# Value tiles in three overlapped steps, later roundings of the weights' sums, and one tile's taps behind x

## The chip, the cores and the metric

The kernel runs on one core of a Trainium2 chip. Such a core has five engines with a queue each: TensorE (PE in the profile; its weight loads are PEld) multiplies, VectorE (DVE), ScalarE (ACT) and GpSimd (POOL) compute elementwise, and SyncE (SP) issues the transfers here. The engines run on their own and meet at semaphores. The metric is the device time of one execution in microseconds, given as the median over runs.

## The reference

Sparse attention feeds a feed-forward block with a convolution gate, which feeds a block with a spatial gate. The change lies at the seam of the last two.

```python
# B, S = 2, 768; 512 model features, 1024 inner features
x = attention(q, k, v)                         # (B, S, 512)

h = np.maximum(x @ w_in, 0.0)                  # first layer
conv_out = sum(conv_w[k] * shifted(h, k - 1) for k in range(3))   # "taps"
gate = 1.0 / (1.0 + np.exp(-conv_out))
x = h * gate @ w_out                           # second layer

h = np.maximum(x @ w_in2, 0.0)                 # third layer
u, v = h[..., :512], h[..., 512:]              # gate halves and value tiles
v_n = (v - mean(v)) / np.sqrt(var(v) + 1e-6)   # over the 512 features of a row
v_s = einsum("ts,bsd->btd", w_spatial, v_n) + b_spatial[None, :, None]
out = (u * v_s) @ w_out2
```

## The kernel before

All products run in fp32 split in two: each operand X is held as a rounded part X_hi and a remainder X_lo = X - X_hi, and each product is three matmuls (hi x hi, hi x lo, lo x hi). ScalarE makes the rounded parts, VectorE the remainders. So nearly every tile that TensorE takes has a rounding on ScalarE and, behind it, a subtraction on VectorE.

The program is written out engine by engine. Each engine's instructions are issued in the order of the code, and a wait on a semaphore holds up everything behind it on that engine. Nothing schedules the work but this order. The stages of the changed stretch, in the order of TensorE's work (b is the batch, 0 or 1; halves c are of the 768 columns):

1. Second layer of batch 0: eight x tiles x2 (`second_layer`), four for each half. Tile n and tile n + 4 share a bank, so TensorE waits for `x2_lo_in` (VectorE's `rest_of_x2(n)`, L1461) before tile n + 4. Beside it VectorE computes taps, gate products and remainders of batch 1: `taps(3, m)` are two operations (L1433, L1438) on tile m of its second half, whose first tap ScalarE has made (L1006).
2. Value tiles of batch 0: six tiles of 128 rows x 512 features (`value_half`), twelve matmuls each, in banks 4 to 7. For tile j ScalarE does `relu_v(j)` (L1044, out of the bank into a ring `vr` of VR = 3 rows), VectorE `row_stats(j)` (L1559, L1561), GpSimd `invert_std(j)` (L842, L845), VectorE `normalise_v(j)` (L1566), ScalarE `round_v(j)` (L1049), VectorE `rest_of_v(j)` (L1572). `relu_v(j)` for j of 3 and more waits for `v_lo_in`, which `rest_of_v(j - 3)` raises. In between ScalarE does sigmoids (L998) and roundings `round_g` (L1003) of batch 1 and VectorE gate products `gate` (L1447).
3. Gate halves of batch 0: eight groups of twelve matmuls (`gate_half`) in banks 0 to 3. ScalarE's `relu_u(n)` (L1055) empties a bank, and TensorE waits for it (`left_u`) before group n + 4.
4. Second layer of batch 1 (`second_layer_by_halves`) in Strassen's form with seven passes of 24 matmuls: X, Y, R, then one that adds onto X (L2139), V, another that adds (L2139), Z. It needs sums of weight blocks (`sum_f2_s`, L1512 to L1520; their roundings `round_f2_s` on ScalarE, L1011; their remainders `rest_of_f2_s` on VectorE, L1527) and differences of activation blocks (`sum_f2_t`, L1495; `rest_of_f2_t`, L1502). X needs g11_lo (L1467); Y needs g21_lo (`rest_of_g21`, L1472); R needs the sum 4 and g22_lo (L1477); the first adding pass needs the sum 2, the difference t2 and "c11" (`sum_f2`, L1548). The differences t overwrite the raw activations, and `rest_of_g21` and what follows write into the place of x2; VectorE therefore waits for `u_done` (all gate halves of batch 0 computed) before `rest_of_g21`.
5. Value tiles and gate halves of batch 1, then the spatial product and the output.

In the second batch VectorE already runs the value tiles as `row_stats(s)`, `normalise_v(s - 1)`, `rest_of_v(s - 2)`; there `vr` has a row for each tile.

Of the kernel before, what the change touches and what calls it, by code (L numbers as in the profile page):

```python
# [15 lines left out]
NT = S // P  # L16
# [5 lines left out]
KD, KF, KH = DM // P, DF // P, DM // P  # L22
# [22 lines left out]
TG = NT // 2  # L45
# [48 lines left out]
FH = KF // 2  # L94
# [30 lines left out]
def build_program(nc, q, k0, k1, v0, v1, n_keys, weights, conv_w, b_spatial, out):  # L125
    ctx = ExitStack()
    with ctx:
# [456 lines left out]
        def f2_t_sum_no(n, f):  # L584
            return FH * F2_T_SUMS.index(n) + f + 1
# [368 lines left out]
        def _(act):  # L954
# [38 lines left out]
            def sigmoid(i):  # L993
                b, c, m, _ = gate_place(i)
                act.wait_ge(tapped, tap_end(2 * b + c, m))
                if b == 1 and c == 0:
                    act.wait_ge(edge_steps, EDGE_STEPS)
                nc.scalar.activation(c_sb[b][c][:, m, :], c_sb[b][c][:, m, :], ACT.Sigmoid).then_inc(sig, 1)  # L998

            def round_g(i):  # L1000
                b, c, m, cols = gate_place(i)
                act.wait_ge(g_raw, i + 1)
                nc.scalar.copy(g_hi[b][c][:, m, :], h_sb[b][:, m, shifted(cols, 1)]).then_inc(g_hi_in, 1)  # L1003
# [36 lines left out]
            def relu_v(i):  # L1040
                act.wait_ge(v_done, i + 1)
                if VR <= i < NT:
                    act.wait_ge(v_lo_in, i + 1 - VR)
                nc.scalar.activation(vr_row(i), banks[4 + i % 4][:], ACT.Relu).then_inc(left_v, 1)  # L1044
# [105 lines left out]

            act.wait_ge(w_split, NW2 + NWI)
            for j in range(NT):
                if j >= 1:
                    round_v(j - 1)
                relu_v(j)
                if j < FH:
                    round_g(2 * KF + FH + j)
                sigmoid(3 * KF + 2 + j)
            round_v(NT - 1)
            for n in range(2 * KH):  # L1160
                relu_u(n)
                if n in (1, 2):
                    for f in range(2):
                        round_g(3 * KF + FH + 2 * (n - 1) + f)
                if n == 3:
                    round_f2_s(4)
                    round_f2_s(2)

# [173 lines left out]
        def _(dve):  # L1344
# [331 lines left out]
                if m in (2, 4):  # L1676
                    split_lo(NW2 + m // 2 - 1)
            rest_of_g(2 * KF - 1)
            for m in range(TG):
                taps(3, m)  # L1680
            for n in range(KD):
                rest_of_x2(n)
            for m in range(TG, KF):
                taps(3, m)
                if m in (TG, TG + 2):
                    split_lo(NW2 + 2 + (m - TG) // 2)
                if m in (TG + 1, TG + 2):
                    rest_of_x2(KD + m - TG - 1)
# [4 lines left out]
            for m in range(FH, KF):  # L1693
                gate(2 * KF + m)
            rest_of_x2(KD + 3)
            for j in range(NT):
                row_stats(j)
                if j >= 1:
                    rest_of_v(j - 1)
                gate(3 * KF + j)  # L1700
                normalise_v(j)
            rest_of_v(NT - 1)
            for m in range(NT, KF):
                gate(3 * KF + m)
            for n in F2_S_SUMS:
                sum_f2_s(n)
            for f in range(FH):
# [1 line left out]
                sum_f2_t(1, f)  # L1709
            for f in range(FH):  # L1710
                sum_f2_t(3, f)
            for n in (4, 2):
                rest_of_f2_s(n)

            dve.wait_ge(u_done, 2 * KH)
            for f in range(FH):
                rest_of_g21(f)
            for f in range(FH):
                sum_f2_t(2, f)
            for f in range(FH):  # L1720
                dve.wait_ge(f2_t_raw, f2_t_sum_no(3, f))
                dve.wait_ge(f2_t_raw, f2_t_sum_no(2, f))
                rest_of_g22(f)
            for f in range(FH):
                sum_f2_t(4, f)
            dve.wait_ge(f2_t_raw, f2_t_sum_no(4, FH - 1))
            rest_of_f2_t(2)
            for i in range(MH):
                sum_f2("c11", i)
# [775 lines left out]
```

## Time and profile before

| | |
|---|---|
| median of 3 runs | 362.48 us (362.22 to 362.89) |
| profiled execution, its own time | 362.81 us |
| its span, first to last instruction | 361.0 us |
| mean clock granted to TensorE | 0.991 of 2.4 GHz |
| busy: TensorE, its weight loads | 97%, 88% |
| busy: VectorE, ScalarE, GpSimd | 73%, 55%, 34% |

The profile is of one execution. Times are in us from the span's start. A line number such as L1055 is a line of the kernel before. Matmuls are pipelined: the records of neighbours overlap, and a busy TensorE is not one at its peak. A timeline row merges several instructions of one form when they follow each other without a gap, and then gives the time of all of them and their count. "Idle before" is time in which the engine had nothing running, with the last semaphore that came in named as what released it. The waits view adds up such idle time. The critical chain of this kernel is TensorE for nearly all of the stretch, so what counts is where TensorE stands still or runs at a lower clock.

### The profile page before, as it was taken

How to read it: one execution, taken by the hardware profiler on the slowest of the kernel's cores; microseconds unless marked ns; L12 is line 12 of the kernel's file. 1: busy time of each engine (PE TensorE's matmuls, PEld its weight loads, DVE VectorE, ACT ScalarE, POOL GpSimd, SP SyncE). 2: the span in 40 equal slices, each digit the busy share in tenths (PEclk: the TensorE clock that was granted, in tenths of full speed). 3: DMA queues.
4: the chain of work that ended last, by engine and by line, in shares of the span. 5: the costliest groups of instructions: out<-in, count | busy, mean ns of one | idle time of the engine just before them, and what ended most of it. 6: DMA issues, size and time to landing. Idle time of an engine off the chain costs nothing. (4 is left out here: it accounts for less than half of the span.)

```text
span 361.0 us, 7513 instructions
## 1 busy us (share of the span) xinstructions
PE 349.3 (97%) x2848; PEld 317.2 (88%) x2849; DVE 264.5 (73%) x618; ACT 200.3 (55%) x491; POOL 124.1 (34%) x191
## 2 busy tenths in 40 slices
PE   8999999999999999999999698999999999999996
PEld 4558898998989999989889698998899999998885
DVE  6996888777885798997556899956885899974000
ACT  4887677776766788794344445734565016314212
POOL 4889896445543003000122100001455570224000
PEclk9999999999999999999999699999999999999999
DMA  7962442333314033300600000004135600001322
GB/s 231 396 221 69 121 130 81 119 98 112 111 46 163 0 118 117 116 2 0 218 17 0 0 3 0 0 2 160 58 118 172 209 1 2 1 0 61 116 88 93
DMA packets 14474, 32.23 MB, mean 89 GB/s; under 512 B 1760, under 2 KB 4832, under 8 KB 14432
## 3 DMA queue, kind: packets, MB, share of 16 engines
q1 hardware_dynamic: 14144, 31.56, 25.7%
q8 instruction: 24, 0.39, 0.5%
q10 hardware_dynamic: 288, 0.13, 0.2%
q14 instruction: 18, 0.15, 0.1%
HBM read 28.54 MB, written 3.15 MB: 88 GB/s over the span
## 5 line engine op out<-in xcount | busy, mean ns | idle before, releaser
L2058 PE MATMUL bank<-xT,w_hi 128*128 128x384 f32 x256 | 69.6, 345 | 0.0
L821 POOL TENSOR_SCALAR p_sb<-p_sb,denom 128x256 f32<-128x256 f32 (+1 forms) x96 | 48.0, 517 | 35.7 <-DVE denom L1408 35.7
L968 ACT ACTIVATE p_sb<-p_sb,row_min 128x256 f32<-128x256 f32 (+1 forms) x96 | 46.3, 487 | 14.9 <-DVE row_min L1397 14.9
L2058 PEld LDWEIGHTS bank<-xT,w_hi 128*128 128x128 f32 x256 | 45.7, 188 | 0.6 <-issue 0.3
L2058 PE MATMUL bank<-xT,w_lo 128*128 128x384 f32 x128 | 44.0, 344 | 0.0
L842 POOL TENSOR_SCALAR rstd<-mean_var 128x1 f32<-128x1 f32 x12 | 5.3, 440 | 105.5 <-DVE mean_var L1561 105.5
L1438 DVE SCALAR_TENSOR_TENSOR c_sb<-h_sb,conv_sb,c_sb 128x382 f32<-128x382 f32 (+2 forms) x56 | 37.3, 666 | 2.0
L1397 DVE CUSTOM_DVE_ANT_0 p_sb<-bank,table 128x256 f32<-128x256 f32 (+1 forms) x96 | 33.0, 398 | 4.9 <-PE bank L1967 4.9
L2013 PE MATMUL bank<-ident,p_sb 128*128 128x128 f32 x176 | 29.3, 281 | 0.8 <-POOL p_sb L821 0.6
L976 ACT COPY pt_sb<-bank 128x512 f32<-128x512 f32 (+1 forms) x44 | 23.9, 544 | 8.5 <-PE bank L2013 8.0
L1062 ACT CAST gt_hi<-gt_raw 128x384 fp32r<-128x384 f32 x16 | 8.2, 514 | 35.8 <-DVE gt_raw L1584 19.4
L2013 PEld LDWEIGHTS bank<-ident,p_sb 128*128 128x128 f32 x176 | 20.3, 140 | 7.5 <-POOL p_sb L821 4.8
L2058 PEld LDWEIGHTS bank<-xT,w_lo 128*128 128x128 f32 x128 | 24.1, 188 | 0.0
L2037 PE MATMUL bank<-pt_sb,v_sb 128*64 128x128 f32 x352 | 23.4, 278 | 0.5 <-DVE pt_sb L1414 0.5
L2037 PEld LDWEIGHTS bank<-pt_sb,v_sb 128*64 128x64 f32 x352 | 18.8, 136 | 5.3 <-issue 3.3
L2102 PE MATMUL bank<-g_hi,w_hi 128*128 128x382 f32 (+1 forms) x64 | 21.8, 340 | 0.6 <-DVE x L1461 0.6
L2104 PE MATMUL bank<-g_hi,w_lo 128*128 128x382 f32 (+1 forms) x64 | 21.6, 338 | 0.0
L2103 PE MATMUL bank<-g_lo,w_hi 128*128 128x382 f32 (+1 forms) x64 | 21.6, 337 | 0.0
L990 ACT ACTIVATE h_sb<-bank 128x384 f32<-128x384 f32 x32 | 15.6, 486 | 10.1 <-PE bank L2058 9.9
L1625 DVE TENSOR_TENSOR w_lo<-stage,w_hi 128x1024 fp32r<-128x1024 f32 (+1 forms) x11 | 16.6, 1506 | 5.5 <-ACT w_hi L962 5.5
L2104 PE MATMUL bank<-w_hi,vn 128*128 128x384 f32 x60 | 20.2, 336 | 0.0
L2102 PE MATMUL bank<-w_hi,vn 128*128 128x384 f32 x60 | 20.2, 336 | 0.0
(213 smaller groups left out, 950.8 us busy)
## 6 DMA issues: line engine op xcount, KB each, us to landing
stage<-in_weights SPq DMA_DIRECT2D x17, 512.0 KB, 3.4
v_sb<-in_v SPq DMA_DIRECT2D x8, 390.0 KB, 3.8
k_sb<-in_k SPq DMA_DIRECT2D x8, 384.0 KB, 4.3
out_dram<-out_sb SPq DMA_DIRECT2D x11, 256.0 KB, 2.0
q_sb<-in_q SPq DMA_DIRECT2D x13, 192.0 KB, 2.4
v_sb<-in_v SPq DMA_DIRECT2D x6, 260.0 KB, 3.9
f_s_raw<-in_weights SPq DMA_DIRECT2D x3, 512.0 KB, 5.9
k_sb<-in_k SPq DMA_DIRECT2D x5, 256.0 KB, 3.7
```

The source lines that it names most:

```text
L821: nc.gpsimd.tensor_scalar(probs_h, probs_h, denom[:, u % SLOTS, h:h + 1], 1.0, ALU.mult, ALU.mult).then_inc(scaled, 1)
L968: nc.scalar.activation(p_sb[:, u % SLOTS, h, 0:n], p_sb[:, u % SLOTS, h, 0:n], ACT.Exp, bias=row_min[:, u % SLOTS, h:h + 1], scale=-1.0, a ...
L976: nc.scalar.copy(pt_sb[:, u % PT_SLOTS, :, 0:n], pt_ps(u)[:, :, 0:n]).then_inc(pt_in, 1)
L1397: nc.vector.tensor_tensor_reduce(out=p_sb[:, u % SLOTS, h, 0:n], in0=score_cols(u, h), in1=table[:, at_col:at_col + n], scale=slope(2 * hp ...
L1438: nc.vector.scalar_tensor_tensor(dst, src, w, dst, ALU.mult, ALU.add).then_inc(tapped, 1)
L1625: nc.vector.tensor_tensor(lo, staged(chunk)[:, 0:hi.shape[-1]], hi.bitcast(F32), ALU.subtract).then_inc(w_split, 1)
L2013: last = nc.tensor.transpose(pt_ps(u)[:, h, c:c + P], p_sb[:, u % SLOTS, h, c:c + P], ident[:])
L2037: last = nc.tensor.matmul(xt_ps[h * D:(h + 1) * D, tt * P:(tt + 1) * P], rows[:, h * DV:h * DV + D], pt_sb[:, u % PT_SLOTS, h, n * P:(n + ...
L2058: last = nc.tensor.matmul(h_bank(j)[:, 0:C], w, x, start=r == 0, stop=r == F1_GROUP - 1)
L2102: nc.tensor.matmul(ps, a_hi, b_hi, start=start, stop=False)
L2103: nc.tensor.matmul(ps, a_hi, b_lo, start=False, stop=False)
L2104: return nc.tensor.matmul(ps, a_lo, b_hi, start=False, stop=stop)
```

## The change

Three things change, all of them by order alone; no instruction is added or taken away.

- **Value tiles of batch 0.** VectorE does two gate products first; then in turn j it does the statistics of tile j, scales tile j - 1, makes the remainder of tile j - 2, and does one gate product. ScalarE does the relu of tile j, a sigmoid and a rounding of g, and then rounds value tile j - 1, where it did that rounding before the relu.
- **Roundings of the weights' sums.** ScalarE's two roundings `round_f2_s(4)` and `(2)` come behind all eight relus of the gate halves (before: behind the fourth), and its four roundings of g22 between those relus come one at a time. VectorE's `rest_of_f2_s(4)` goes from before the wait for `u_done` to behind `sum_f2_t(2, ...)`, and `rest_of_f2_s(2)` to just before `rest_of_f2_t(2)`.
- **Taps.** VectorE does the taps of two tiles instead of three (TG is 3) before the first four `rest_of_x2`; the third tile's come behind them.

```diff
--- before.py
+++ after.py
@@ -1150,21 +1150,19 @@
 
             act.wait_ge(w_split, NW2 + NWI)
             for j in range(NT):
+                relu_v(j)
+                sigmoid(3 * KF + 2 + j)
+                if j < FH:
+                    round_g(2 * KF + FH + j)
                 if j >= 1:
                     round_v(j - 1)
-                relu_v(j)
-                if j < FH:
-                    round_g(2 * KF + FH + j)
-                sigmoid(3 * KF + 2 + j)
             round_v(NT - 1)
             for n in range(2 * KH):
                 relu_u(n)
-                if n in (1, 2):
-                    for f in range(2):
-                        round_g(3 * KF + FH + 2 * (n - 1) + f)
-                if n == 3:
-                    round_f2_s(4)
-                    round_f2_s(2)
+                if 1 <= n <= FH:
+                    round_g(3 * KF + FH + n - 1)
+            round_f2_s(4)
+            round_f2_s(2)
 
 
 
@@ -1676,11 +1674,11 @@
                 if m in (2, 4):
                     split_lo(NW2 + m // 2 - 1)
             rest_of_g(2 * KF - 1)
-            for m in range(TG):
+            for m in range(2):
                 taps(3, m)
             for n in range(KD):
                 rest_of_x2(n)
-            for m in range(TG, KF):
+            for m in range(2, KF):
                 taps(3, m)
                 if m in (TG, TG + 2):
                     split_lo(NW2 + 2 + (m - TG) // 2)
@@ -1693,15 +1691,17 @@
             for m in range(FH, KF):
                 gate(2 * KF + m)
             rest_of_x2(KD + 3)
-            for j in range(NT):
-                row_stats(j)
-                if j >= 1:
-                    rest_of_v(j - 1)
-                gate(3 * KF + j)
-                normalise_v(j)
-            rest_of_v(NT - 1)
-            for m in range(NT, KF):
+            for m in range(2):
                 gate(3 * KF + m)
+            for j in range(NT + 2):
+                if j < NT:
+                    row_stats(j)
+                if 1 <= j <= NT:
+                    normalise_v(j - 1)
+                if j >= 2:
+                    rest_of_v(j - 2)
+                if j < NT:
+                    gate(3 * KF + 2 + j)
             for n in F2_S_SUMS:
                 sum_f2_s(n)
             for f in range(FH):
@@ -1709,14 +1709,13 @@
                 sum_f2_t(1, f)
             for f in range(FH):
                 sum_f2_t(3, f)
-            for n in (4, 2):
-                rest_of_f2_s(n)
 
             dve.wait_ge(u_done, 2 * KH)
             for f in range(FH):
                 rest_of_g21(f)
             for f in range(FH):
                 sum_f2_t(2, f)
+            rest_of_f2_s(4)
             for f in range(FH):
                 dve.wait_ge(f2_t_raw, f2_t_sum_no(3, f))
                 dve.wait_ge(f2_t_raw, f2_t_sum_no(2, f))
@@ -1724,6 +1723,7 @@
             for f in range(FH):
                 sum_f2_t(4, f)
             dve.wait_ge(f2_t_raw, f2_t_sum_no(4, FH - 1))
+            rest_of_f2_s(2)
             rest_of_f2_t(2)
             for i in range(MH):
                 sum_f2("c11", i)
```

Behind the edit on ScalarE the line numbers of the changed kernel are lower by 2: L1566 is L1564, for instance.

VectorE around the x tiles of batch 0, before: behind the last remainders of g come pairs of taps (into c_sb_84), then the four remainders of x.

```order
L1453 TENSOR_TENSOR g_lo_79<-h_sb_77,g_hi_86 128x386 x2
L1433 SCALAR_TENSOR_TENSOR c_sb_84<-h_sb_78,conv_sb,c_sb_84 128x384
L1438 SCALAR_TENSOR_TENSOR c_sb_84<-h_sb_78,conv_sb,c_sb_84 128x384
L1433 SCALAR_TENSOR_TENSOR c_sb_84<-h_sb_78,conv_sb,c_sb_84 128x384
L1438 SCALAR_TENSOR_TENSOR c_sb_84<-h_sb_78,conv_sb,c_sb_84 128x384
L1433 SCALAR_TENSOR_TENSOR c_sb_84<-h_sb_78,conv_sb,c_sb_84 128x384
L1438 SCALAR_TENSOR_TENSOR c_sb_84<-h_sb_78,conv_sb,c_sb_84 128x384
L1461 TENSOR_TENSOR x_76<-bank,x_76 128x382 x4
```

After:

```order
L1451 TENSOR_TENSOR g_lo_79<-h_sb_77,g_hi_86 128x386 x2
L1431 SCALAR_TENSOR_TENSOR c_sb_84<-h_sb_78,conv_sb,c_sb_84 128x384
L1436 SCALAR_TENSOR_TENSOR c_sb_84<-h_sb_78,conv_sb,c_sb_84 128x384
L1431 SCALAR_TENSOR_TENSOR c_sb_84<-h_sb_78,conv_sb,c_sb_84 128x384
L1436 SCALAR_TENSOR_TENSOR c_sb_84<-h_sb_78,conv_sb,c_sb_84 128x384
L1459 TENSOR_TENSOR x_76<-bank,x_76 128x382 x4
L1431 SCALAR_TENSOR_TENSOR c_sb_84<-h_sb_78,conv_sb,c_sb_84 128x384
L1436 SCALAR_TENSOR_TENSOR c_sb_84<-h_sb_78,conv_sb,c_sb_84 128x384
```

One pair of taps, of the third tile, has moved behind the remainders of x.

ScalarE in the value tiles of batch 0, before, two turns in the middle: L1049 rounds a value tile, L1044 is the relu of the next.

```order
L1049 CAST vn_90<-vr_97 128x512
L1044 ACTIVATE vr_97<-bank 128x512
L1003 CAST g_hi_87<-h_sb_78 128x384
L998 ACTIVATE c_sb_84<-c_sb_84 128x384
L1049 CAST vn_90<-vr_97 128x512
L1044 ACTIVATE vr_97<-bank 128x512
L1003 CAST g_hi_87<-h_sb_78 128x384
```

After:

```order
L1049 CAST vn_90<-vr_97 128x512
L1044 ACTIVATE vr_97<-bank 128x512
L998 ACTIVATE c_sb_84<-c_sb_84 128x384
L1003 CAST g_hi_87<-h_sb_78 128x384
L1049 CAST vn_90<-vr_97 128x512
L1044 ACTIVATE vr_97<-bank 128x512
L998 ACTIVATE c_sb_84<-c_sb_84 128x384
```

The rounding of the value tile stood first in a turn, ahead of the relu; now it is the turn's last and belongs to the tile before.

VectorE in the same turns, before: statistics of tile j, remainder of tile j - 1, a gate product, scaling of tile j.

```order
L1559 BN_STATS stats<-vr_97 128x6
L1561 BN_AGGR mean_var<-stats 128x2
L1572 TENSOR_TENSOR vn_90<-vr_97,vn_90 128x512
L1447 TENSOR_TENSOR h_sb_78<-c_sb_84,h_sb_78 128x384
L1566 TENSOR_SCALAR vr_97<-vr_97,mean_var,rstd 128x512
L1559 BN_STATS stats<-vr_97 128x6
```

After:

```order
L1557 BN_STATS stats<-vr_97 128x6
L1559 BN_AGGR mean_var<-stats 128x2
L1564 TENSOR_SCALAR vr_97<-vr_97,mean_var,rstd 128x512
L1570 TENSOR_TENSOR vn_90<-vr_97,vn_90 128x512
L1445 TENSOR_TENSOR h_sb_78<-c_sb_84,h_sb_78 128x384
L1557 BN_STATS stats<-vr_97 128x6
```

The statistics and the aggregate now have the scaling of the tile before right behind them, and the remainder is of the tile before that.

VectorE from the differences t to the first "c11" in the second layer of batch 1, before (f_s_lo are the remainders of the weights' sums, g_lo with h_sb_78,g_hi_87 those of g21, g_lo_80 those of g22).

```order
L1495 TENSOR_TENSOR h_sb_78<-h_sb_78 128x384 x5
L1527 TENSOR_TENSOR f_s_lo<-f_s_raw,f_s_hi 128x1024 x2
L1472 TENSOR_TENSOR g_lo<-h_sb_78,g_hi_87 128x384 x4
L1495 TENSOR_TENSOR f_t_raw<-h_sb_78 128x384 x4
L1477 TENSOR_TENSOR g_lo_80<-h_sb_78,g_hi_88 128x384 x4
L1495 TENSOR_TENSOR h_sb_78<-h_sb_78,f_t_raw 128x384 x4
L1502 TENSOR_TENSOR f_t_lo<-f_t_raw,f_t_hi 128x384 x4
L1548 TENSOR_TENSOR f_y_125<-bank,f_y_125 128x384
```

After:

```order
L1493 TENSOR_TENSOR h_sb_78<-h_sb_78 128x384 x5
L1470 TENSOR_TENSOR g_lo<-h_sb_78,g_hi_87 128x384 x4
L1493 TENSOR_TENSOR f_t_raw<-h_sb_78 128x384 x4
L1525 TENSOR_TENSOR f_s_lo<-f_s_raw,f_s_hi 128x1024
L1475 TENSOR_TENSOR g_lo_80<-h_sb_78,g_hi_88 128x384 x4
L1493 TENSOR_TENSOR h_sb_78<-h_sb_78,f_t_raw 128x384 x4
L1525 TENSOR_TENSOR f_s_lo<-f_s_raw,f_s_hi 128x1024
L1500 TENSOR_TENSOR f_t_lo<-f_t_raw,f_t_hi 128x384 x4
L1546 TENSOR_TENSOR f_y_125<-bank,f_y_125 128x384
```

The two f_s_lo, neighbours ahead of the g21 remainders before, now stand one behind the differences t2 (f_t_raw) and one behind the differences t4 (h_sb_78<-h_sb_78,f_t_raw).

## Rows read from the trace of the kernel before

**Rows 1.** waits of TensorE: engine line waited for: us in total, times, longest

```profile
PE bank L2102 <- ACT u_sb L1055: 3.6, 1, 3.6
...
PE bank L2141 <- DVE g_lo L1472: 1.3, 1, 1.3
```

**Rows 2.** timeline of TensorE: start us, us, engine line op out<-in xcount [idle before <-releaser]

```profile
156.27 0.45 PE L2102 MATMUL bank<-g_hi,w_hi 128*128 128x386 f32 x1 [0.65 <-DVE x L1461]
```

**Rows 3.** page, part 2: clock granted to TensorE in 40 slices of the span

```profile
PEclk9999999999999999999999699999999999999999
```

**Rows 4.** windows: stretch, length, busy by engine (count), PEclk, DMA share, GB/s

```profile
201.90:207.80 5.90, 5.90 (x19) 5.90 (x20) 5.80 (x7) 2.72 (x7) 0.00 (x0) 0.51 0.00 0
```

**Rows 5.** timeline of TensorE, gate halves to second layer

```profile
201.89 0.69 PE L2102 MATMUL bank<-x,wi_hi 128*128 128x384 f32 x1 [3.61 <-ACT u_sb L1055]
...
207.78 0.34 PE L2102 MATMUL bank<-x,wi_hi 128*128 128x384 f32 x1
...
213.01 0.34 PE L2141 MATMUL bank<-g_hi,w_hi 128*128 128x384 f32 x1
```

**Rows 6.** timeline of ScalarE, relus of value tiles and of gate halves

```profile
176.43 0.60 ACT L1044 ACTIVATE vr<-bank 128x512 f32<-128x512 f32 x1 [2.27 <-PE bank L2104]
...
180.35 0.59 ACT L1044 ACTIVATE vr<-bank 128x512 f32<-128x512 f32 x1
...
201.35 0.87 ACT L1055 ACTIVATE u_sb<-bank 128x384 f32<-128x384 f32 x2
```

**Rows 7.** timeline of TensorE, first value tile and first gate half

```profile
173.41 0.40 PE L2102 MATMUL bank<-wi_hi,x 128*128 128x512 f32 x1
...
189.77 0.33 PE L2102 MATMUL bank<-x,wi_hi 128*128 128x384 f32 x1
```

**Rows 8.** timeline of VectorE, one value tile

```profile
180.98 0.69 DVE L1559 BATCH_NORM_STATS2 stats<-vr 128x6 f32<-128x512 f32 x1 [1.18 <-ACT vr L1044]
181.77 0.18 DVE L1561 BATCH_NORM_AGGREGATE mean_var<-stats 128x2 f32<-128x6 f32 x1
181.87 0.66 DVE L1572 TENSOR_TENSOR vn<-vr,vn 128x512 fp32r<-128x512 f32 x1
...
183.45 0.55 DVE L1566 TENSOR_SCALAR vr<-vr,mean_var,rstd 128x512 f32<-128x512 f32 x1 [0.45 <-POOL rstd L845]
```

**Rows 9.** timeline of VectorE, a scaling in the second batch

```profile
253.85 0.52 DVE L1566 TENSOR_SCALAR vr<-vr,mean_var,rstd 128x512 f32<-128x512 f32 x1
```

**Rows 10.** timeline of VectorE, weights' sums to the second layer

```profile
203.02 1.22 DVE L1512 TENSOR_TENSOR w_lo_raw<-f_s_raw,w_lo_raw 128x1024 f32<-128x1024 f32 x1
...
207.94 0.55 DVE L1467 TENSOR_TENSOR g_lo<-h_sb,g_hi 128x384 fp32r<-128x384 f32 x1
...
214.35 2.35 DVE L1527 TENSOR_TENSOR f_s_lo<-f_s_raw,f_s_hi 128x1024 fp32r<-128x1024 f32 x2
...
216.62 1.95 DVE L1472 TENSOR_TENSOR g_lo<-h_sb,g_hi 128x384 fp32r<-128x384 f32 x4
...
237.83 0.56 DVE L1548 TENSOR_TENSOR xq_raw<-bank,f_v 128x384 f32<-128x384 f32 x1 [0.94 <-PE bank L2139]
```

**Rows 11.** timeline of TensorE, Y pass and first adding pass

```profile
218.62 0.44 PE L2141 MATMUL bank<-g_hi,w_hi 128*128 128x384 f32 x1 [1.28 <-DVE g_lo L1472]
...
218.90 0.34 PE L2141 MATMUL bank<-g_lo,w_hi 128*128 128x384 f32 x1
...
227.15 0.33 PE L2139 MATMUL bank<-f_t_hi,f_s_hi 128*128 128x384 f32 x1
```

**Rows 12.** timelines of ScalarE and VectorE around the x tiles

```profile
154.15 2.05 ACT L1037 ACTIVATE x<-bank 128x382 fp32r<-128x382 f32 x4
...
154.48 0.61 DVE L1433 SCALAR_TENSOR_TENSOR c_sb<-h_sb,conv_sb,c_sb 128x384 f32<-128x384 f32 x1
...
155.67 1.93 DVE L1461 TENSOR_TENSOR x<-bank,x 128x382 fp32r<-128x382 f32 x4
...
161.68 0.56 DVE L1461 TENSOR_TENSOR x<-bank,x 128x386 fp32r<-128x386 f32 x1 [0.58 <-ACT x L1037]
```

## The prediction

> **What bounds the kernel now.** Times are microseconds from the span's start. I read the waits of TensorE first: after the start-up it stops for others three times that matter, 3.6 us for the relu of a gate half (L1055) and 1.3 us for a remainder of the gated activations (L1472) [rows 1], and 0.65 us for the remainder of an x tile (L1461) [rows 2]. Elsewhere in the changed stretch it goes from matmul to matmul, so these stops, and what hangs on them, are all that the change can win. The clock row [rows 3] is full but for one place, and the window over it [rows 4] says 0.51 of 2.4 GHz, the lower level, from 201.9 to 207.8, directly after the 3.6 us stop. The record of a 384-column matmul lasts 0.34 us while the next starts 0.174 us after it (207.78 to 213.01 is 30 matmuls [rows 5]), so a stop of x idle us sets TensorE back by x + 0.17.
>
> Why the long stop is there shows in the timelines. ScalarE's relu of a value tile comes every 4.2 us (180.35 to 201.35 is five turns) [rows 6], while TensorE makes a tile in 2.73 (173.41 to 189.77 is six) [rows 7]. The turn is a round trip: relu 180.35, statistics 180.98, then VectorE stands still until GpSimd's root is in and scales the rows at 183.45 [rows 8], then ScalarE's copy of the rounded value, and only then the next relu. The last copy holds up the first relu of the gate halves until 201.35, and TensorE needs that bank.
>
> **Part 1, the value tiles in three steps.** ScalarE now does relu(j), sigmoid, rounding and only then round_v(j-1); VectorE does row_stats(j), normalise_v(j-1), rest_of_v(j-2), a gate product. No instruction is added. The trip to GpSimd falls into the time in which the next tile is computed, as it does in the second batch, where the scaling starts without idle time [rows 9]. What can still close a loop is the ring of three rows: relu(j) waits for rest_of_v(j-3). Its length: relu to statistics 0.63 (180.35 to 180.98), statistics and aggregate 0.89 (180.98 to 181.87), scaling 0.47 (0.55 less the 0.08 by which two records overlap), remainder 0.66 [rows 6, 8], start of the relu 0.03: 2.68, against TensorE's 2.73. The gate product of about 0.55 fits into the 0.63. So I take it that each relu follows its tile by the 0.1 of the first one: tile 0 ends at 173.41 + 11 x 0.227 + 0.39 = 176.30, its relu is at 176.43 [rows 6], and the sixth is at about 190.03 instead of 197.15.
>
> From there on: statistics from 190.66, aggregate ended 191.63, the root 1.50 later (181.95 to 183.45 [rows 8]) at 193.13, scaling 0.55, copy of the last row from 193.71, ScalarE free at 194.24, first gate relu ended at 194.72. TensorE wants it after 48 matmuls from 189.77, at 198.12: cover of 3.4 us. **The stop goes: 3.61 + 0.17 = 3.78 us.** With it goes what the half clock followed upon: 18 matmuls from 201.89 to 207.78 took 5.89 [rows 5] where 18 x 0.174 = 3.13 would do. **2.76 us.**
>
> **Part 2, what VectorE then has to do.** Call U the start of the second layer's first pass (213.01 [rows 5]; new 189.77 + 96 x 0.174 = 206.47). VectorE has its last value remainder behind it at 194.97, then four weight sums 4.92 (203.02 to 207.94) and twelve remainders and differences 6.41 (207.94 to 214.35) [rows 10]: 206.30. It then waits for u_done, until U + 0.17 + 0.04 = 206.68. That wait cost nothing before (VectorE came at 214.35, after the last gate matmul); now it holds VectorE 0.4 us, and all of the following queue stands behind it. One 384-wide operation takes a place of 0.467 (four are 1.95, one 0.55), a 1024-wide one 1.14 (214.35 to 216.62 is two) [rows 10].
> - The two f_s_lo remainders (L1527, 2.27 us) move from ahead of the g21 remainders to behind. g21 ends at U + 0.21 + 3 x 0.467 + 0.55 = U + 2.16; the Y pass wants it at U + 24 x 0.174 = U + 4.18. **The stop goes: 1.28 + 0.17 and the slow restart (0.28 for a place of 0.174 [rows 11]) are 1.56 us.** Nothing is late there for 2 us more.
> - f_s_lo(4) ends at about U + 5.1 and g22 at U + 0.21 + 8 x 0.467 + 1.14 + 1.40 + 0.55 = U + 7.0; the R pass wants both at U + 8.4.
> - f_s_lo(2), four remainders of t2 and c11 are wanted by the first adding pass (L2139). It came at 227.15, which is 8.42 after Y began at the full rate (218.90 - 0.17) [rows 11], so it is due at U + 4.18 + 8.42 = U + 12.60. VectorE: 0.21 + 16 x 0.467 + 1.14 + 0.12 (f_s_lo(2) waits for the difference just before it; 0 to 0.2) + 1.14 + 4 x 0.467 + 0.56 = U + 12.5. Cover 0.1 us or none: here the change makes a new tight place. Nothing can be won by it; above, 0.25. **I take 0.1 lost.**
> - Behind it VectorE is 0.4 us later against TensorE than before, until it next waits for it (0.94 idle at 237.83 [rows 10]); that takes it up.
>
> ScalarE: its roundings of the sums now stand behind all eight gate relus and run from U + 0.65 to U + 2.7; VectorE asks for the first at U + 3.95. The four g roundings, one behind each of the gate relus 1 to 4, are out near 201.5 and asked for at U + 5.1 = 211.6. The DMAs of the sums' inputs hang on x2_done and come as before.
>
> **Part 3, one tile's taps behind x.** VectorE did the taps of tile 2 from 154.48 to 155.67 and only then the first remainder of x, though ScalarE's rounding of it began at 154.15 and takes about 0.5 (four are 2.05) [rows 12]. New: start 154.67, end 155.22. TensorE's next matmul was due 0.65 + 0.17 before 156.27 [rows 2], at 155.45: no stop. **0.65 + 0.17 + 0.10 (a restart as above) = 0.92 us.** VectorE now follows ScalarE's roundings (four in 2.05, the last ends 156.20), so its further taps come some 0.4 us later than before; the 0.58 us that it sits idle before 161.68 [rows 12] cover that. The 0.92 shifts everything after it alike, and no cover above depends on it.
>
> **Sum.** 0.92 + 3.78 + 2.76 + 1.56 - 0.10 = 8.92. The profiled run took 362.81 (span 361.0 and 1.8 around it): 353.9. The median of the three runs is 0.33 lower: 353.6.
>
> **Rivals.**
> 1. *VectorE becomes the bound at the adding pass.* The ring's loop is not 2.68 but longer, between that and the 4.2 of now. At 3.2 the three tiles that wait for the ring are 1.4 late, 0.4 of it vanishes in the wait for u_done and 0.9 comes out at the adding pass: 354.5. At 4.2 they are 4.4 late: gate stop 1.0, Y 1.0, adding pass 1.8: 357.4. For: the slack is 0.05 a tile. Against: every piece of the loop has a row. 0.13.
> 2. *The clock.* The half-clock stretch is not the stop's doing and comes all the same: 2.8 us stay, 356.4. For: TensorE would run without a break from before 156 on, which no row shows. Against: it fell at the only long stop and was full in the busy stretches around it [rows 3]. 0.04.
> 3. *Slower: VectorE's queue between u_done and c11*, 22 operations packed without a gap, each taking its place longer; the adding pass waits for all of it. The nearest longer place is that of an operation that reads what the one before wrote: of the 6.41 us for twelve, eight are 8 x 0.467, and the four that read cost 0.67. At 0.2 more each it is 4.4 us, 358.0; the kernel is slower only from 8.92 / 22 = 0.41 more each, and at 0.45 it takes 363.5. Against: the same operations stand in fours of 1.95 [rows 10]. 0.02. The Trainium skill (VectorE: DVE Perf Modes, The DRAIN you can't avoid) says that the next operation does not start until the pipe is empty, a drain of roughly the duration less 266 ns. By that a place would be 0.55 + 0.28 = 0.83 us and the queue some 9 us longer, which would leave about 362.6. This trace does not agree: a place is 0.467 [rows 10].
> 4. *Part 3 does nothing*, since ScalarE's rounding and not the taps ends last: 354.5. ScalarE's row says otherwise. 0.05.
>
> **Numbers.** The forecast has 0.76. Range 353.0 to 355.6: the forecast with its unknowns and the spread of the runs (0.6 below), rival 4, and rival 1 up to a loop of some 3.5; about 0.1 is left out. About 0.2% (0.7 us) is what can be told from no change: faster 0.96, same 0.02, slower 0.02.
>
> **What would show it.** TensorE's waits lose L1055, L1472 and L1461; its clock row has no dip; relus of value tiles every 2.73; the second layer's first pass at about 205.5; a wait at the first adding pass of at most 0.25. A turn over 2.8 would show rival 1, a half clock without a stop rival 2, places over 0.5 in VectorE's queue rival 3, a stop near 155.5 rival 4. The forecast is wrong if a DMA or GpSimd becomes the last to arrive anywhere between 150 and 245.

## The result, and the profile after

The changed kernel takes 353.31 us, the median of four runs (353.14 to 353.42), where the kernel before, run beside it, takes 362.6 (four runs, 362.22 to 362.89). The ratio is 0.974, 95% interval 0.973 to 0.976: faster by 9.3 us. The forecast was 353.6. The profiled execution after took 353.42 us with a span of 351.6; before they were 362.81 and 361.0.

The waits of TensorE over the whole span of the kernel after (engine line waited for: us in total, times, longest) and its clock row (40 slices, tenths of full speed):

```profile
PE bank L2069 <- POOL zeros L782: 1.3, 1, 1.3
PE bank L1967 <- DMA k_sb<-in_k: 0.9, 1, 0.9
PE bank L2013 <- POOL p_sb L821: 0.6, 2, 0.4
PE bank L2037 <- DVE pt_sb L1412: 0.5, 3, 0.2
PE bank L2065 <- issue: 0.2, 1, 0.2
```

```profile
PEclk9999999999999999999999999999999999999999
```

Only the waits of the attention at the start are left. The three stops of [rows 1, 2] are gone, and so is the dip in the clock row [rows 3]. The window over the changed stretch (busy time of PE, PEld, DVE, ACT and POOL, then the clock) has TensorE busy in all of it:

```profile
155.00:240.00 85.00, 85.00 (x458) 81.10 (x457) 72.63 (x134) 47.80 (x97) 7.40 (x13) 1.00 0.10 35
```

TensorE's timeline at the places that the prediction speaks of (start, duration):

```profile
155.32 0.34 PE L2104 MATMUL bank<-g_hi,w_lo 128*128 128x382 f32 x1
155.50 0.34 PE L2102 MATMUL bank<-g_hi,w_hi 128*128 128x386 f32 x1
...
188.89 0.33 PE L2102 MATMUL bank<-x,wi_hi 128*128 128x384 f32 x1
...
205.56 0.34 PE L2141 MATMUL bank<-g_hi,w_hi 128*128 128x384 f32 x1
...
209.72 0.33 PE L2141 MATMUL bank<-g_hi,w_hi 128*128 128x384 f32 x1
...
218.23 0.41 PE L2139 MATMUL bank<-f_t_hi,f_s_hi 128*128 128x384 f32 x1
```

The second half of x now follows its neighbour at 155.50, by the usual 0.17 us, where it stood at 156.27 [rows 2]. The gate halves start at 188.89 (189.77, [rows 7]), the second layer's X pass at 205.56 (213.01, [rows 5]), its Y pass at 209.72 (218.62) and the first adding pass at 218.23 (227.15, [rows 11]). Against its own work TensorE gained like this:

| stretch of TensorE | before | after | gained | forecast |
|---|---|---|---|---|
| span's start to first gate half | 189.77 | 188.89 | 0.88 | 0.92 |
| first gate half to X | 23.24 | 16.67 | 6.57 | 6.54 |
| X to R | 9.93 | 8.38 | 1.55 | 1.56 |
| R to the first adding pass | 4.21 | 4.29 | -0.08 | -0.10 |
| adding pass to V | 4.18 | 4.24 | -0.06 | 0 |
| V to the last matmul | 125.93 | 125.93 | 0.00 | 0 |
| behind the last matmul's start | 3.74 | 3.20 | 0.54 | 0 |

ScalarE's relus of value tiles and first of the gate halves, from its timeline after:

```profile
175.55 0.60 ACT L1044 ACTIVATE vr<-bank 128x512 f32<-128x512 f32 x1 [2.27 <-PE bank L2104]
...
180.93 0.60 ACT L1044 ACTIVATE vr<-bank 128x512 f32<-128x512 f32 x1
...
183.67 0.60 ACT L1044 ACTIVATE vr<-bank 128x512 f32<-128x512 f32 x1
...
189.15 0.60 ACT L1044 ACTIVATE vr<-bank 128x512 f32<-128x512 f32 x1
...
193.34 0.87 ACT L1055 ACTIVATE u_sb<-bank 128x384 f32<-128x384 f32 x2
```

Six relus in five turns of 2.72 us on average, where a turn took 4.2 [rows 6]. The sixth starts at 189.15; the forecast was 190.03 less the 0.87 that all work had come forward, 189.16. The first gate relu ends at 193.83, and TensorE comes for its bank at 188.89 + 48 x 0.1736 = 197.22: the cover is 3.4 us, as forecast.

VectorE in one turn of the value loop, at the first of the weights' sums, and then from its wait for `u_done` to "c11":

```profile
184.30 0.69 DVE L1557 BATCH_NORM_STATS2 stats<-vr 128x6 f32<-128x512 f32 x1 [0.26 <-ACT vr L1044]
185.10 0.18 DVE L1559 BATCH_NORM_AGGREGATE mean_var<-stats 128x2 f32<-128x6 f32 x1
185.20 0.52 DVE L1564 TENSOR_SCALAR vr<-vr,mean_var,rstd 128x512 f32<-128x512 f32 x1
185.63 0.69 DVE L1570 TENSOR_TENSOR vn<-vr,vn 128x512 fp32r<-128x512 f32 x1
186.23 0.55 DVE L1445 TENSOR_TENSOR h_sb<-c_sb,h_sb 128x384 f32<-128x384 f32 x1
187.04 0.69 DVE L1557 BATCH_NORM_STATS2 stats<-vr 128x6 f32<-128x512 f32 x1 [0.26 <-ACT vr L1044]
...
194.08 1.22 DVE L1510 TENSOR_TENSOR w_lo_raw<-f_s_raw,w_lo_raw 128x1024 f32<-128x1024 f32 x1
...
205.76 1.97 DVE L1470 TENSOR_TENSOR g_lo<-h_sb,g_hi 128x384 fp32r<-128x384 f32 x4 [0.28 <-PE bank L2104]
...
209.52 1.22 DVE L1525 TENSOR_TENSOR f_s_lo<-f_s_raw,f_s_hi 128x1024 fp32r<-128x1024 f32 x1
...
214.52 1.23 DVE L1525 TENSOR_TENSOR f_s_lo<-f_s_raw,f_s_hi 128x1024 fp32r<-128x1024 f32 x1
215.66 1.96 DVE L1500 TENSOR_TENSOR f_t_lo<-f_t_raw,f_t_hi 128x384 fp32r<-128x384 f32 x4
217.54 1.01 DVE L1546 TENSOR_TENSOR f_y<-bank,f_y 128x384 f32<-128x384 f32 x2
```

No scaling (L1564) has an idle time in front of it, where GpSimd's root held it up for 0.45 in [rows 8]. The wait for `u_done` is now 0.28 us of idle time (0.4 forecast). The first half of c11 ends at 217.54 + 0.55 = 218.09, which is X + 12.53 (forecast 12.5), and the adding pass starts at X + 12.67 with a first record of 0.41 us in place of 0.34 and 0.25 to the next: the new tight place is there, at a price of 0.08.

### The profile page after: what moved, and what is told of

The parts are those of the page before. It is cut to its first block, busy times and chain, and to the rows that moved or that the text cites. A ratio compares the mean times of both kernels' runs of the same rounds, so it can differ in the third digit from the quotient of the medians.

```text
span 351.6 us, 7512 instructions
## 1 busy us (share of the span) xinstructions
PE 345.0 (98%) x2848; PEld 313.9 (89%) x2849; DVE 263.8 (75%) x618; ACT 201.1 (57%) x491; POOL 124.4 (35%) x191
## 4 chain that ended last, share of the span: by engine, by line
PE 86%; DVE 6%; POOL 5%; issue 1%; DMA 1%; ACT 1%; DVEq 0%; ACTq 0%
PE bank L2102 16%; PE bank L2104 16%; PE bank L2103 16%; PE bank L2058 16%; PE bank L2141 6%; PE bank L2037 4%; PE bank L2013 4%; PE bank L2262 3%; PE bank L2139 2%; POOL p_sb L821 2%; PE bank L1967 2%; DVE p_sb L1395 2%; POOL w_lo L838 1%; DMA counts<-in_n_keys 1%; DVE denom L1404 1%
## 5 line engine op out<-in xcount | busy, mean ns | idle before, releaser
L842 POOL TENSOR_SCALAR rstd<-mean_var 128x1 f32<-128x1 f32 x12 | 4.5, 379 | 96.8 <-DVE mean_var L1559 96.8
```

## The experiments

Ratios below are to the kernel before, from the runs made beside each; "X", "Y", "R" and "adding pass" are TensorE's starts. The kernel before takes times in two groups (see the last section): its median was 363.58 us beside the first four experiments below (19 runs), 362.21 beside the next three sections (7 runs) and 362.62 beside the longer turn (7 runs). A ratio of one section is therefore not to be set against that of another; the readings below rest on the traces and on the kernels' own times.

### Part 1 alone

```diff
             for j in range(NT):
+                relu_v(j)
+                sigmoid(3 * KF + 2 + j)
+                if j < FH:
+                    round_g(2 * KF + FH + j)
                 if j >= 1:
                     round_v(j - 1)
...
+            for j in range(NT + 2):
+                if j < NT:
+                    row_stats(j)
+                if 1 <= j <= NT:
+                    normalise_v(j - 1)
+                if j >= 2:
+                    rest_of_v(j - 2)
```

The kernel before with the new order of the value tiles on both engines, and nothing else.

> The kernel before with part 1 alone: the three-step order of the value tiles on ScalarE and VectorE, nothing else. Theory: the gate stop (3.78) and the half clock behind it (2.76) go, and the stop at the Y pass goes too without any move of the weights' sums, because VectorE now comes 8 us earlier to the two f_s_lo remainders: they run 206.3 to 208.6, g21 ends at 210.5 and Y is due at 210.65. So all but part 3 is won: 362.6 - 8.2 = about 354.4 to 354.1, no wait on L1472. Rival: the Y stop needs the move of the sums (part 2); then 1.56 us stay, about 355.7, with a wait of 1.3 us on L1472.

Measured: 354.13 us (353.78 to 354.80), ratio 0.974 (0.971 to 0.976), span 352.4. TensorE's waits from 150 on in this kernel:

```profile
PE bank L2104 <- DVE x L1461: 0.7, 1, 0.7
```

The stop of 3.6 us, the half clock and also the 1.3 us stop at Y are gone. The two f_s_lo remainders still stand ahead of the g21 remainders on VectorE:

```profile
206.23 2.35 DVE L1527 TENSOR_TENSOR f_s_lo<-f_s_raw,f_s_hi 128x1024 fp32r<-128x1024 f32 x2
208.50 1.96 DVE L1472 TENSOR_TENSOR g_lo<-h_sb,g_hi 128x384 fp32r<-128x384 f32 x4
```

The g21 remainders end at 210.46, and TensorE starts Y at 210.56, 24 matmuls behind X (206.40). So part 2 is not needed to remove the stop at Y.

### Part 3 alone

```diff
-            for m in range(TG):
+            for m in range(2):
                 taps(3, m)
             for n in range(KD):
                 rest_of_x2(n)
-            for m in range(TG, KF):
+            for m in range(2, KF):
```

> The kernel before with part 3 alone: one tile's taps behind the x remainders. Theory: the x stop (0.65 + 0.17 + restart 0.1, in the changed kernel 0.87 by the start of the value tiles, 173.41 to 172.54) goes, and since the later stops are round trips that start with TensorE's own value tiles they shift with it: 361.7. Rival: the later 3.6 us stop ends at its own time and swallows the gain: 362.6, with that stop at 4.5 instead of 3.6 us.

Measured: 361.58 us (361.09 to 363.28), ratio 0.996 (0.994 to 0.998). The stop before the second half of x is gone (155.28), the value tiles start at 172.30 instead of 173.41, and the stops of 3.6 and 1.2 us stay. This part does what it says, by itself and with the others.

### Part 2 alone

```diff
-            for n in (4, 2):
-                rest_of_f2_s(n)
 
             dve.wait_ge(u_done, 2 * KH)
...
+            rest_of_f2_s(4)
...
+            rest_of_f2_s(2)
             rest_of_f2_t(2)
```

With the roundings on ScalarE behind the gate relus, as in the change.

> The kernel before with part 2 alone: roundings of the weights' sums behind the gate relus, f_s_lo remainders behind u_done. Theory: the Y stop (1.56) goes, but VectorE's queue up to c11 is as long as before (c11 ends at 226.7) while the adding pass is now due at 225.6, so about 1.0 comes back there: 362.1, with a new wait of about 1 us at L2139. Rival: no wait at the adding pass, 361.0; or nothing, 362.6.

Measured: 362.09 us (361.47 to 362.35), ratio 0.996 (0.994 to 0.998). TensorE's waits from 150 on:

```profile
PE bank L2100 <- ACT u_sb L1055: 3.6, 1, 3.6
PE bank L2137 <- DVE f_y L1546: 1.1, 1, 1.1
PE bank L2100 <- DVE x L1459: 0.6, 1, 0.6
```

The Y stop goes, and 1.05 of it comes back at the first adding pass, which starts at 226.91 in place of 227.15. VectorE's queue is as long as before and merely in another order, so what is wanted last in it is as late as before.

### Parts 1 and 3 without part 2

The changed kernel with the roundings and remainders of the weights' sums back in their old places (the lines of the last diff reversed).

> The changed kernel without part 2 (the weights' sums as before). Theory: part 2 is worth nothing once part 1 is there; it only moves 2.27 us of VectorE work from a place with 0.1 us of cover at Y to one with none at the adding pass, which costs 0.08 there: 353.2 to 353.4, equal to the changed kernel's 353.3, c11 with about 0.4 us of cover. Rival: without part 2 the Y stop returns, 354.8.

Measured: 353.50 us (353.0 to 353.9), ratio 0.972 (0.970 to 0.974), span 351.3. TensorE has no wait behind 150, X is at 205.36 and the adding pass at 218.00, X + 12.64, against X + 12.67 in the changed kernel. Here c11 starts at 216.96 and its first half ends 0.5 us ahead of the adding pass. **Part 2 is worth nothing once part 1 is there.** It moves cover: without it the last g21 remainder ends 0.1 us ahead of Y (209.42 against 209.53) and 0.5 are left at the adding pass; with it there are 2.0 at Y (207.73 against 209.72) and none at the adding pass.

### ScalarE's half of part 1 without VectorE's

```diff
-            for j in range(NT + 2):
+            for j in range(NT):
                 row_stats(j)
+                if j >= 1:
+                    rest_of_v(j - 1)
+                gate(3 * KF + j)
+                normalise_v(j)
```

The changed kernel with VectorE's loop of before: it waits for GpSimd's root again.

> The changed kernel with VectorE's value loop as it was (statistics, remainder of j-1, gate product, scaling of j) and only ScalarE's order new. Theory: it is ScalarE's order that opens the round trip; VectorE still stands still for GpSimd's root, 2.47 from statistics to scaling and 0.47 for the scaling, so its turn is 2.94 instead of 2.74, no more than 1.1 late after five turns, and two gate products (0.94) come behind the loop. The gate stop stays away (3.4 us of cover); VectorE reaches u_done about 1.2 late and the adding pass waits for that: 354.5, with relus of value tiles at 2.73. Rival: both halves are needed, the turn stays near 4.2 and the gate stop returns: 357 or more.

Measured: 354.24 us (353.84 to 354.67), ratio 0.978 (0.974 to 0.981). The waits on the root are back on VectorE, and this is all that TensorE sees of them:

```profile
189.38 0.55 DVE L1564 TENSOR_SCALAR vr<-vr,mean_var,rstd 128x512 f32<-128x512 f32 x1 [0.44 <-POOL rstd L845]
```

```profile
218.86 0.41 PE L2137 MATMUL bank<-f_t_hi,f_s_hi 128*128 128x384 f32 x1 [0.84 <-DVE f_y L1546]
```

The relus come every 2.71 us (175.26 to 188.80) and there is no gate stop. So nearly all of part 1's gain comes from ScalarE's order: that it takes relu(j) before round_v(j-1). VectorE's order is worth 0.9 us here (the adding pass is at X + 13.59 against X + 12.67). The other half by itself was not tried: with ScalarE rounding tile j-1 before relu(j), and VectorE taking the statistics of j before the scaling of j-1, each would wait for the other.

### A stop of 2 us, and one of 4

```diff
             round_v(NT - 1)
+            for k in range(10):
+                nc.scalar.copy(zeros[:, 0:C], x2[:, 0, 0, 0:C].bitcast(F32)).then_inc(extra, 1)
+                act.wait_ge(extra, k + 1)
             for n in range(2 * KH):
                 relu_u(n)
```

The changed kernel with ScalarE held up ahead of the gate relus; the second kernel has 13 copies. This prices the stop and the clock apart from the value tiles.

> The changed kernel with ten extra 384-wide copies on ScalarE (each waiting for the one before, so about 0.55 to 0.6 each) ahead of the gate relus. They use up the 3.4 us of cover and make TensorE stop about 2.2 us at the fifth gate half. Theory: a stop costs its length and 0.2, the clock stays at the upper level: 353.3 + 2.5 = 355.8. Rival: any stop at this place brings the half clock: 2.8 more, 358.6.

> The same with thirteen extra copies: a stop of about 3.8 us at the same place as in the kernel before. Theory: the half clock is the stop's doing, so it comes back: 353.3 + 3.9 + 0.2 + 2.8 = 360.2, granted clock near 0.5 for some 6 us behind the stop. Rival: the half clock had another cause that the change took away; then 357.4 and a full clock.

The first took 355.99 us (355.90 to 357.13), ratio 0.983 (0.980 to 0.987). In its profiled execution the clock stays full, and the matmul behind the stop is followed after 0.28 us, the ones after it after 0.17 to 0.19:

```profile
199.14 0.45 PE L2106 MATMUL bank<-x,wi_hi 128*128 128x384 f32 x1 [1.99 <-ACT u_sb L1056]
199.42 0.34 PE L2107 MATMUL bank<-x,wi_hi 128*128 128x384 f32 x1
```

First gate half to X is 18.96 us against 16.67: 2.29 = 1.99 + 0.17 + some 0.1 for the restart, the prices that the prediction used. One of the four runs was longer than the rest: 357.13 us at a mean clock of 0.995, where the others took 355.90 to 356.03 at 1.000. It has no trace; its clock says that the half clock probably did follow the stop there, so the rival may hold in one run of four.

The second took 358.85 us (358.41 to 359.56), ratio 0.990 (0.987 to 0.993). It has the stop of the kernel before, 3.62 us, and the clock falls behind it:

```profile
201.19 0.44 PE L2106 MATMUL bank<-x,wi_hi 128*128 128x384 f32 x1 [3.62 <-ACT u_sb L1056]
...
201.85 0.52 PE L2106 MATMUL bank<-x,wi_hi 128*128 128x384 f32 x1
202.17 0.52 PE L2107 MATMUL bank<-x,wi_hi 128*128 128x384 f32 x1
...
205.29 0.33 PE L2108 MATMUL bank<-x,wi_lo 128*128 128x384 f32 x1
```

From 201.19 to 205.29 are 14 matmuls in 4.10 us, 2.44 at full rate: 1.66 lost, restart included, where [rows 5] lose 2.76. The half clock follows the stop, as the theory had it, but stops of 3.61 and 3.62 us are followed by half clocks of different length. That is most of the miss of 1.35 us against the time expected; the stop was also 0.3 us shorter than the 3.9 put in.

### VectorE's queue longer by 1.2 us

```diff
             dve.wait_ge(u_done, 2 * KH)
+            for _ in range(2):
+                extra_add()
             for f in range(FH):
                 rest_of_g21(f)
```

`extra_add` is an addition of 384 columns into unused memory that VectorE waits for. The two took 1.19 us.

> The changed kernel with two extra 384-wide additions on VectorE right behind its wait for u_done (each waits for the one before, 0.65 each, 1.3 in all). Theory: the adding pass is the tight place, with no cover, so all of it comes out there and nothing at Y (2 us of cover): 353.3 + 1.3 = 354.6, waits of about 1.2 us at L2139 and at most 0.1 at the R pass. Rival: there is cover elsewhere in VectorE's queue and the time stays at 353.3 to 353.6.

Measured: 354.33 us (354.26 to 355.25), ratio 0.978 (0.975 to 0.982).

```profile
219.06 0.41 PE L2150 MATMUL bank<-f_t_hi,f_s_hi 128*128 128x384 f32 x1 [1.03 <-DVE f_y L1547]
```

The adding pass is at X + 13.86, 1.19 later than in the changed kernel; Y and R don't move. So this place has no cover at all, and VectorE's time there goes to TensorE one for one.

### A longer turn of the value loop

```diff
                 if 1 <= j <= NT:
                     normalise_v(j - 1)
+                if 1 <= j < NT:
+                    extra_add()
                 if j >= 2:
                     rest_of_v(j - 2)
```

> The changed kernel with one more VectorE addition (384 columns, waiting for itself, about 0.65 us) in every turn of the loop over value tiles. It prices the first rival of the prediction. By the prediction's reading VectorE waits in that loop of the changed kernel while the first turns are paced by ScalarE (turns of 2.7 us, VectorE idle for 0.3 to 1.4 us in each), so the first addition or two are hidden; then the ring through VectorE becomes the bound, turns grow to about 3.3 us, and the relus of tiles 3 to 5 end about 1.8 us late in all. The gate's rounding has 3.4 us of cover, so TensorE doesn't stop there, and the start of the second layer's first pass stays where it is in the changed kernel (within 0.3). VectorE comes to its wait for the gate's values some 1.8 us later; it had idled there a few tenths, so its queue is about 1.5 us late at the second adding pass, where TensorE then waits about 1.0 us: 354.5 to 354.9 us. The rival: the ring is no bound even so (TensorE's start to the end unchanged, 353.3), or the delay reaches the gate as well (a stop there of over 1 us, and 356 or more).

Measured: 355.84 us (355.49 to 356.14), ratio 0.979 (0.976 to 0.983). One turn of the ring, on ScalarE and on VectorE:

```profile
184.31 0.60 ACT L1045 ACTIVATE vr<-bank 128x512 f32<-128x512 f32 x1 [0.64 <-DVE vn L1571]
...
187.65 0.60 ACT L1045 ACTIVATE vr<-bank 128x512 f32<-128x512 f32 x1 [0.64 <-DVE vn L1571]
```

```profile
184.95 0.69 DVE L1558 BATCH_NORM_STATS2 stats<-vr 128x6 f32<-128x512 f32 x1 [0.26 <-ACT vr L1045]
...
186.27 0.56 DVE L1631 TENSOR_TENSOR stage<-h_sb 128x384 f32<-128x384 f32 x1
186.86 0.69 DVE L1571 TENSOR_TENSOR vn<-vr,vn 128x512 fp32r<-128x512 f32 x1
```

The ring is the bound now: a turn is 3.34 us, of which the addition has 0.59. Without it the loop is 2.75, just over TensorE's 2.73; the prediction put it together as 2.68 (the remainder's end to the relu's start is 0.10 us and not 0.03). The relus of tiles 3 to 5 are 1.83 us late in all (189.15 to 190.98), as priced, and then VectorE's queue is another 0.5 us later, since the last turn, in which no relu waits any more, has its addition too; the expectation forgot that one. The sums start 2.36 us later (194.08 to 196.44). The delay comes out at four places, restarts included: 0.2 us at X (205.80), 0.2 at Y (210.12), 0.8 at R (215.10, a stop of 0.50 for the g22 remainders) and 1.2 at the adding pass (a stop of 1.03), in all 2.35 us there (218.23 to 220.58) and at the last matmul. The time lies 0.9 us above the range expected.

### Both kernels once more

> The kernel before once more, for the stretch behind TensorE's last matmul: from that matmul's start to the end of the span was 3.74 us in its first profile, against 3.20 in the changed kernel's, and the last issue of the output on SP's queue took 1.20 us against 0.51. If this half microsecond belongs to the run and not to the kernel, the stretch comes out somewhere between 3.2 and 3.7 us here, and the issue somewhere between 0.3 and 1.2. If it belongs to the kernel before, 3.7 and 1.2 come again.

> The changed kernel once more, for the same stretch: if the half microsecond belongs to the kernel, 3.20 us and an issue of 0.51 us come again; if it belongs to the run, they come out anywhere between 3.2 and 3.7 us, and 0.3 and 1.2. TensorE's start to its last matmul should be 348.4 us within 0.1 either way.

Behind the last matmul's start the kernel before now has 3.37 us (3.74 the first time) and the changed one 3.68 (3.20); the last issue on SP's queue took 0.33 us in the kernel before (1.20 the first time) and 1.17 in the changed one (0.51). The 0.54 us of the table is therefore the profiled execution's and not the kernel's. The changed kernel's last matmul is at 348.42 again (348.40).

The kernel before showed something else: its last matmul is at 358.83 and not at 357.26. Its clock row and two windows of 9 us (clock in the third column from the end, behind the five engines):

```profile
PEclk9999999999999999999999898999999999999999
```

```profile
200.00:209.00 9.00, 7.09 (x32) 7.10 (x33) 7.85 (x10) 4.72 (x10) 0.23 (x1) 0.81 0.00 0
218.00:227.00 9.00, 8.36 (x39) 8.36 (x40) 8.97 (x20) 4.64 (x11) 0.00 (x0) 0.81 0.00 0
```

and its timeline of TensorE at the two stops:

```profile
201.91 0.67 PE L2102 MATMUL bank<-x,wi_hi 128*128 128x384 f32 x1 [3.62 <-ACT u_sb L1055]
...
205.49 0.33 PE L2104 MATMUL bank<-x,wi_lo 128*128 128x384 f32 x1
...
212.04 0.42 PE L2141 MATMUL bank<-g_hi,w_hi 128*128 128x384 f32 x1
...
218.64 0.45 PE L2141 MATMUL bank<-g_hi,w_hi 128*128 128x384 f32 x1 [2.15 <-DVE g_lo L1472]
...
219.14 0.52 PE L2141 MATMUL bank<-g_hi,w_lo 128*128 128x384 f32 x1
```

The half clock behind the first stop lasts 3.6 us in place of 5.9, and X starts 0.97 us earlier (212.04 against 213.01). Nothing is won by it: Y starts at 218.64, where [rows 11] have 218.62, since VectorE reaches the g21 remainders at 216.63 either way (216.62 in [rows 10]). The stop there is 2.15 us instead of 1.28, the clock falls a second time behind it, and that costs the 1.57 us.

## Why the prediction was right, and where its account was not

**The total.** 0.92 + 3.78 + 2.76 + 1.56 - 0.10 = 8.92 was forecast for TensorE and 8.86 came (357.26 to 348.40). Every stretch of the table up to the last matmul is within 0.06 us of its term. The forecast of 353.6 lies 0.3 from the median. The last 0.54 us of the difference in span, behind the last matmul, was not forecast and doesn't belong to the change.

**Part 1** did what the prediction said, by the mechanism that it named: the round trip of 4.2 us is taken apart, the relus come every 2.66 to 2.74 us at TensorE's pace of 2.73, and the gate stop goes with the half clock behind it. The kernel with the longer turn shows how close rival 1 was: the loop is 2.75 where 2.68 was worked out and 2.73 is TensorE's pace. The last three turns of the changed kernel, 2.74 each (180.93 to 189.15), already go by the ring: with VectorE's old loop, where the relus wait for TensorE, they are 2.72. It costs nothing at 0.02 us a turn. What the prediction didn't separate is which engine's order does it. It is ScalarE's; VectorE's adds 0.9 us.

**The Y stop was put to the wrong part.** The prediction credited 1.56 us to the move of the f_s_lo remainders. Part 1 alone removes the stop, and without part 2 the time is the same (353.50 and 353.31, and the adding pass at X + 12.64 and X + 12.67). The step that failed is the one that took the order at Y as the cause of the lateness there. In the kernel before VectorE last stood still at the last remainder of a value tile:

```profile
201.47 0.69 DVE L1572 TENSOR_TENSOR vn<-vr,vn 128x512 fp32r<-128x512 f32 x1 [0.68 <-ACT vn L1049]
```

From there it waited for no other engine until 237.83 [rows 10]: it was late at Y because it had left the value tiles late. Part 1 alone brings it to the weights' sums 8.11 us earlier (203.02 to 194.91), and with part 3 it is 8.94 (203.02 to 194.08), which is the gain of the kernel, 8.86, within 0.1. Had the prediction worked out Y with part 1 alone (from 194.97: sums 4.92, remainders and differences 6.41, the two f_s_lo remainders 2.27, the g21 remainders 1.95: 210.5 against 210.7), it would have seen that nothing is late there.

**The terms of the clock and of Y are one.** 2.76 for the half clock and 1.56 for Y were summed as if each could be had alone. The second profile of the kernel before shows that what the one gives back the other takes: with the half clock's loss down to 1.67 us, X came 0.97 earlier and the stop at Y grew by 0.87. The 19 runs of that kernel beside the first experiments say the same: of the nine between 361.9 and 362.7 us, three have a mean clock of 0.995 (the short fall) and six one of 0.990 or 0.991 (the long one, as in the profile ahead of the prediction), and the times are alike: 361.99 to 362.59 and 361.92 to 362.74. The sum was right because part 1 takes away both causes at once, the stop of TensorE and the lateness of VectorE.

**The new tight place** came as forecast, 0.08 for 0.10, and with no cover; VectorE reaches the end of c11 at X + 12.53 where 12.5 was worked out. It is the work of part 2, and without part 2 there are 0.5 us of cover.

**Part 3** gave 0.87 for 0.92; rival 4 is out. **Rival 2** is out: TensorE runs from 155 to 240 without a break at a clock of 1.00. **Rival 3** is out for the places: four operations of 384 columns take 1.95 to 1.97 us in the new order as in the old one. The Trainium skill (VectorE: DVE Perf Modes, The DRAIN you can't avoid) has each operation wait for the one before it to drain, but adds that a next operation that is not held starts earlier; the prediction left this out when it said that the trace disagrees. The rows agree with that addition: 0.467 us from one start to the next, for a duration of 0.55. An addition followed by a wait for it took a place of 0.59.

**Open.** Why the half clock behind the same stop lasts 5.9 us in one execution and 3.6 in another. Two profiles of one kernel show both, so the program alone doesn't set it; nothing that was run tells what does.

## What to carry to other kernels

When one engine stands still for another, follow that other engine back to its last idle time before an order near the stop is blamed: if its queue is packed from there on, a reorder only moves the stop to whatever is wanted last, and the cause lies where the queue starts. Stops that share such a late engine are one term of the sum and not several. Where two engines take turns on a tile through a third, the order that puts the next tile's first step ahead of this tile's last one is worth the most on the engine that frees the bank.

## What was not expected of the hardware

**One stop, several prices.** Behind a stop of 3.6 us the granted clock fell to the lower level (1.2 GHz) in all five profiles that had it, but TensorE lost 2.8 us by it in the first profile of the kernel before, 2.9 with part 3 alone, 2.5 with part 2 alone, and 1.7 in the second profile of the kernel before and in the kernel with 13 copies. Behind a stop of 2.15 us it fell too, for a loss of 1.57; behind one of 1.99 us, in another kernel, it did not fall in the profile (one of four runs of that kernel was 1.1 us longer, at a mean clock of 0.995), nor behind those of 1.28 us and less.

**The kernel before has two times.** The 19 runs beside the first experiments lie at 361.9 to 362.7 (9 of them) and at 363.6 to 364.6 (10), with nothing between; of all 39 executions on record 23 are at 362.89 or less and 16 at 363.58 or more. The profiled execution at 362.81 has one fall of the clock, the one at 363.98 has two, and their last matmuls are 1.57 us apart. The upper group has a mean clock of 0.990 or 0.991 in all ten, which is what two short falls give. That the second fall makes this group is shown for the one profile and argued for the rest. The kernel with part 2 alone speaks for it: it keeps the first stop but has none at Y, and none of its eight runs, made beside the 19, lies above 362.35. The changed kernel (353.1 to 353.9 in five executions) and the one without part 2 (353.0 to 353.9 in five) have no stop in this stretch, a clock of 0.999 or 1.000 and no second group. So beside a run of the upper group (its middle is at 364.07) the change is worth about 1.5 us more than the 9.3 of the four runs; that none of the four, nor the profile that the prediction started from, was one is chance.
